# Fused top-32 attention and Mish feed-forward block on one core: another order of the work inside a slot on ScalarE and GpSimd, and the w_out split moved from slots 0 to 3 to slots 3 to 6

## The reference

```python
scores = q @ k.T / 8                       # per batch and head, 576 x 576
kth    = np.partition(scores, -32)[..., -32]
attn   = softmax(where(scores >= kth, scores, -1e9))
x      = (attn @ v) as 2304 x 512
h      = x @ w_in                          # 512 x 2048
g      = h * tanh(log1p(exp(h)))           # Mish
y      = g @ w_out                         # 2048 x 512
```

## Time and profile before

| | |
|---|---|
| median of 3 runs | 836.46 us (835.62 to 837.28) |
| profiled execution, its own time | 834.65 us |
| its span, first to last instruction | 832.9 us |
| mean granted TensorE clock | 0.975 of full |
| TensorE busy | 739.1 us (89%) |
| VectorE busy | 702.5 us (84%) |
| ScalarE busy | 557.2 us (67%) |
| GpSimd busy | 552.3 us (66%) |

### The profile page before, as it was taken

The page is one execution under the profiler, slowest core; times in us unless marked ns, Lnnn a source line. Parts: engine busy times, 40 slices in busy tenths (PEclk is TensorE's granted clock), DMA queues, the critical chain, the costliest instruction groups (busy, mean ns, idle before and its releaser), DMA issues.

```text
span 832.9 us, 16813 instructions
## 1 busy us (share of the span) xinstructions
PE 739.1 (89%) x6352; PEld 656.0 (79%) x6352; DVE 702.5 (84%) x1513; ACT 557.2 (67%) x994; POOL 552.3 (66%) x679
## 2 busy tenths in 40 slices
PE   2136787998999999999999999998999999999998
PEld 2125786887898888888888888888898888888896
DVE  5568999997999999989999999969999999996000
ACT  3456577686777686868686868685858686867330
POOL 3487556778676767787776767677676676767233
PEclk9995799999999999999999999999999999999999
DMA  7630000011020000111110000010110000000000
GB/s 225 241 106 7 7 11 4 20 43 42 14 71 8 21 15 16 27 41 48 39 35 8 20 8 23 14 48 8 36 51 18 10 21 7 17 1 14 2 13 25
DMA packets 27858, 28.87 MB, mean 35 GB/s; under 512 B 2433, under 2 KB 20865, under 8 KB 27265
## 3 DMA queue, kind: packets, MB, share of 16 engines
q1 hardware_dynamic: 27776, 27.80, 10.5%
HBM read 23.07 MB, written 4.72 MB: 33 GB/s over the span
## 4 chain that ended last, share of the span: by engine, by line
PE 61%; POOL 15%; ACT 9%; DVE 8%; issue 4%; DMA 2%; SPq 1%; ACTq 0%
PE ps_u L328 26%; PE ps_y L341 17%; POOL p_sb L564 7%; PE ps_s L289 7%; PE ps_o L312 6%; PE ps_s L275 5%; DVE left L507 3%; DVE top L515 3%; POOL w_lo L539 2%; ACT pT L419 2%; POOL g_lo L550 2%; ACT x_sb L394 2%; ACT p_sb L402 1%; DMA g_raw<-w_out 1%; POOL k_lo L528 1%
## 5 line engine op out<-in xcount | busy, mean ns | idle before, releaser
L515 DVE MAX8 top<-left 128x8 f32<-128x576 f32 x432 | 303.8, 745 | 0.0
L328 PE MATMUL ps_u<-xT,win 128*128 128x128 f32 x2304 | 280.2, 281 | 18.3 <-ACT xT L427 18.2
L328 PEld LDWEIGHTS ps_u<-xT,win 128*128 128x128 f32 x2304 | 267.9, 195 | 30.2 <-ACT xT L427 21.2
L564 POOL TENSOR_TENSOR p_sb<-x_sb,p_sb 128x576 f32<-128x576 f32 x144 | 201.7, 1423 | 84.5 <-ACT p_sb L402 84.4
L507 DVE MATCH_REPLACE8 left<-top,left 128x576 f32<-128x576 f32 x288 | 211.6, 742 | 0.0
L410 ACT ACTIVATE p_sb<-p_sb,neg_max 128x576 f32<-128x576 f32 x144 | 111.5, 774 | 84.4 <-POOL p_sb L564 84.2
L419 ACT ACTIVATE pT<-ps_s 128x640 f32<-128x640 f32 x144 | 93.8, 702 | 93.7 <-PE ps_s L289 93.2
L289 PE MATMUL ps_s<-ident,p_sb 128*128 128x128 f32 x720 | 95.3, 282 | 30.0 <-ACT x_sb L394 30.0
L341 PE MATMUL ps_y<-w_hi,g_hi 128*128 128x512 f32 x288 | 118.8, 412 | 0.7 <-ACT y_sb L450 0.7
L402 ACT ACTIVATE p_sb<-x_sb,limit 128x576 f32<-128x576 f32 x144 | 103.8, 775 | 22.8 <-POOL limit L555 22.8
L341 PE MATMUL ps_y<-w_hi,g_lo 128*128 128x512 f32 x288 | 112.6, 391 | 0.0
(11 more groups left out here) (38 smaller groups left out, 718.8 us busy)
## 6 DMA issues: line engine op xcount, KB each, us to landing
k_raw<-k_in SPq DMA_DIRECT2D x16, 288.0 KB, 3.2
q_raw<-q_in SPq DMA_DIRECT2D x64, 64.0 KB, 1.8
v_sb<-v_in SPq DMA_DIRECT2D x16, 256.0 KB, 2.9
win<-w_in SPq DMA_DIRECT2D x4, 1024.0 KB, 7.9
g_raw<-w_out SPq DMA_DIRECT2D x8, 512.0 KB, 3.8
y_out<-y_sb SPq DMA_DIRECT2D x16, 256.0 KB, 2.0
q_raw<-q_in SPq DMA_DIRECT2D x8, 128.0 KB, 2.0
v_sb<-v_in SPq DMA_DIRECT2D x16, 32.0 KB, 3.0
```

Of the source, the lines that this page charges most:

```text
L328: mm = pe.matmul(ps_u[:, n % 2, i, :], win[:, k, P * f:P * f + P], xT[:, k, :], start=(k == 0), stop=(k == KC - 1), skip_group_check=True)
L515: dve.max(best[:, t, EIGHT * r + EIGHT:EIGHT * r + 2 * EIGHT], left[:, t, :]).then_inc(found, 1)
L564: pool.tensor_tensor(p, x_sb[:, s % XS, t, :], p, ALU.subtract).then_inc(arg_ready, 1)
```

## The change

On ScalarE `copy_xT`, `copy_x` and `copy_y` go ahead of `exps` in a slot. On GpSimd the splits of keys and queries leave the end of slot s and go into slot s+1, behind `guard`, `negate` and `split_g` and ahead of `exponents`. The `w_out` split (ScalarE, GpSimd) and its loads (SyncE) move three slots later, to slots 3 to 6. Pairs 0 to 3 are split in slots -3, -2, -1 and 0, one a slot.

```diff
-WCHUNKS = 8
+WCHUNKS, WSLOT = 8, 3
...
-SPLIT_SLOT = {g: max(-3, g - 4) if g < PPB else LAST_USE[g - PPB] - 2 for g in range(PAIRS)}
+SPLIT_SLOT = {g: g - 3 if g < PPB else LAST_USE[g - PPB] - 2 for g in range(PAIRS)}
...
 # SyncE
-                if 1 <= s < WCHUNKS // 2:
-                    load_w(2 * s)
-                    load_w(2 * s + 1)
+                if 1 <= s - WSLOT < WCHUNKS // 2:
+                    load_w(2 * (s - WSLOT))
+                    load_w(2 * (s - WSLOT) + 1)
...
 # ScalarE
-                if 0 <= s - LAG_EXP < DUOS:
-                    exps(s - LAG_EXP)
-                m, j = divmod(s - DOWN_SLOT, GROUPS)
-                if m >= 0 and j == GROUPS - 1:
-                    copy_y(m)
                 if s >= LAG_PT and (s - LAG_PT) % PPB == PPB - 1:
                     copy_xT((s - LAG_PT) // PPB)
                 if 0 <= s + 2 < DUOS:
                     copy_x(s + 2)
+                m, j = divmod(s - DOWN_SLOT, GROUPS)
+                if m >= 0 and j == GROUPS - 1:
+                    copy_y(m)
+                if 0 <= s - LAG_EXP < DUOS:
+                    exps(s - LAG_EXP)
                 for g in splits_at(s):
                     split_k(g)
                 if s + 3 < DUOS:
                     split_q(s + 3)
-                if 0 <= s < WCHUNKS // 2:
-                    split_w(2 * s)
-                    split_w(2 * s + 1)
+                if 0 <= s - WSLOT < WCHUNKS // 2:
+                    split_w(2 * (s - WSLOT))
+                    split_w(2 * (s - WSLOT) + 1)
...
 # GpSimd
+            def splits(s):
+                for g in splits_at(s):
+                    split_k(g)
+                if s + 3 < DUOS:
+                    split_q(s + 3)
+
             for s in range(-3, DUOS + LAG_NORM):
+                if s == -2:
+                    splits(-3)
                 if 0 <= s - LAG_NORM:
                     guard(s - LAG_NORM)
                 if 0 <= s - LAG_EXP < DUOS:
...
                 m, j = divmod(s - MISH_SLOT - 1, GROUPS)
                 if m >= 0 and j < 2:
                     split_g(m, j)
+                if s > -2:
+                    splits(s - 1)
                 if 0 <= s - LAG_EXP < DUOS:
                     exponents(s - LAG_EXP)
                 if 0 <= s - LAG_NORM:
                     normalise(s - LAG_NORM)
-                for g in splits_at(s):
-                    split_k(g)
-                if s + 3 < DUOS:
-                    split_q(s + 3)
-                if 0 <= s < WCHUNKS // 2:
-                    split_w(2 * s)
-                    split_w(2 * s + 1)
+                if 0 <= s - WSLOT < WCHUNKS // 2:
+                    split_w(2 * (s - WSLOT))
+                    split_w(2 * (s - WSLOT) + 1)
```

## The result

The changed kernel takes 839.36 us (median of 6 runs, 838.77 to 840.6) against 835.66 us for the kernel before (6 runs, 833.73 to 837.28) on the same chips: a ratio of 1.0046, 95% interval 1.0031 to 1.0062. It is slower by half a per cent. The forecast was 833.8 us, range 823 to 841: the time lies in the range, on the other side of no change. The profiled execution took 840.6 us, the slowest of the six, with a span of 838.8 us, 5.9 more than before; between the medians it is 3.7.

The account below looks back on a forecast made before the run. VectorE was taken to bound up to slot 12, TensorE from there. 12.9 + 0.3 + 10.9 + 2.9 - 11.7 - 2.2 - 7.5 - 3.0 = 2.6 us gained: median 833.8 us, range 823 to 841.

Parts of the forecast that it names:

- Start, +12.9 and +0.3: Top-k start up to slot 8 gains 12.9 us; the road from limit(10) to TensorE's slot 12 gains 0.3.
- The ring of a slot with the w_out split: VectorE slot with w_out split, limit to next limit: 12.0 us taken; four such slots cost 7 us in all.
- The late load that I had priced: load_w queued behind a load_q waiting for the later q_lo; 0.8 us more for each slot it hits.
- xT, +10.9: TensorE's 0.9 us wait of up for xT goes in 12 slots from 18 to 66: 10.9 us gained.
- slot 70, +2.9: Wait for xT of 1.84 us and half clock behind it shrink to some 0.7: 2.9 us gained.
- q_lo in regular blocks, -11.7: Scores wait 0.58 and 0.48 us for q_lo behind split_g, 11 times in slots 19 to 68: 11.7 us lost.
- Slots with keys, -2.2 and -7.5: k_lo behind split_g delays q_lo: 2.2 us lost net in slots 30 to 32, 7.5 in the two mixed blocks.
- The clock, -3.0: TensorE falls to half clock after two of four new waits of 3.5 us or more: 3.0 us lost.
- rival B: Clock falls after all four long waits and in slot 11: 4.5 us more lost, 838.3 us; chance 0.22.
- C: Chain over mish, split_g and q_lo longer by 0.4 us in 28 slots: 11 us lost, 845 us; chance 0.20.
- D: ScalarE or GpSimd gets ahead, q_lo never late in regular blocks; the 11.7 us stay, 822 us; chance 0.10.

Follow-up runs that it names:

- the kernel with late keys: Changed kernel with splits of keys and queries ahead of split_g, but keys behind normalise in slots with s mod 4 = 0: 804.52 us, ratio 0.963.
- The filled kernel: Changed kernel with 15 to 30 transposes of the identity after values in slots 11, 15, 16, 31, 51 and 52: 833.66 us, ratio 0.9977.
- the kernel with GpSimd's old order: Changed kernel with GpSimd's splits back at the end of slot s, ScalarE's order new: 818.21 us, ratio 0.9797.
- the kernel with `q_lo` first: Changed kernel with GpSimd's splits of keys and queries moved ahead of split_g: 813.11 us, ratio 0.9728.

## Why the prediction was wrong

The forecast was 2.6 us of gain; between the profiled executions it is a loss of 5.9, so 8.5 are missing. The medians miss by less (839.4 for 833.8), since the profiled execution of the changed kernel is its slowest.

**Start, +12.9 and +0.3.** Right in kind; it gave 11.3 up to slot 8 and 9.6 up to slot 12. Two terms were mis-sized. The ring of a slot with the w_out split I put at 12.0 for all four; the later ones took 11.8, but the first took 14.3 (limit at 38.26, then at 52.56). Its scores, which ScalarE now awaits ahead of `exps`, came 3.0 us late; the later the load of queries shown above landed in the four profiles, the later slot 8 began. The late load that I had priced was one of w_out. So the stall came four times and not three in this execution; the kernel with late keys has three. And the road from top-k of slot 11 to slot 12 took 11.3 instead of 9.3: scores and `up` of slot 11 ran at half clock, 2.1 us. The filled kernel, where they do not, has slot 11 shorter by 0.7.

**xT, +10.9, and slot 70, +2.9.** Right: no wait for xT between slots 10 and 70, which gave 11.1, and slot 70 gave 2.8. Slots 14 and 50 gave 0.7 that I had not counted.

**q_lo in regular blocks, -11.7.** Right in place and mechanism. Slots with s mod 4 = 3 lost 0.58, as added up; those with s mod 4 = 0 lost 0.72 instead of 0.48. The 22 slots lost 14.1. Part of this is one gap that was too short: the table load ahead of `exps` starts only when `copy_y`, 0.61, has ended, where I had 0.48.

```profile
266.85 0.61 ACT L450 ACTIVATE y_sb<-ps_y 128x512 f32<-128x512 f32 x1
267.47 1.28 ACT L410 ACT_TABLE_LOAD   x1
```

**Slots with keys, -2.2 and -7.5.** The waits alone were near: 4.71 for 4.87 in slot 15, 2.35 for 2.55 in slot 31. Those of slots 16, 52 and 32 were smaller than forecast (2.56 and 2.64 for 3.55, 0.96 for 1.88), since half clock in `up` of the slot before runs while GpSimd works on. The filled kernel bears this out: with `up` at full clock, scores of slot 16 come 3.8 us late and those of slot 32 2.1.

**The clock, -3.0.** This is the step that failed, and it turned the sign. I took half clock for two of four long waits. It followed all four, and also the waits of slot 11, which only rival B had, and of slot 31, whose wait was forecast, but with no fall behind it. Scores and `up` in these six slots ran 11.5 us longer than at full clock: 2.1 in slot 11, 1.6 in 31, 2.5 and 1.5 in the first mixed block, 2.4 and 1.5 in the second (the 10.6 in the expectation above took 1.94 for scores at full clock, where it is 1.70). About 3 of these are given back by the smaller waits just named. Slots 15 to 17 thus cost 7.2 us against before, not 4.5, and slots 51 to 53 5.8, not 3.05 (the half clock of slot 53, 1.5, is gone, as forecast); slots 31 to 33 cost 2.9, not 2.2. The three numbers of the forecast leave out its 3.0 for the clock. So half clock cost about 8 us where 3.0 were allowed. The filled kernel shows the cause by experiment: 5.7 us back between medians, with 2.6 still lost in slot 32. That brings it to 0.9977 of the kernel before (0.9963 to 0.999), the side of the forecast. Since 1.2 us of the gain in its profile lie at the start, where nothing was changed, how much of the 5.7 is the clock stays open by about that.

Rival B had this mechanism and 838.3 us; I gave it 0.22. That the median of 839.4 is so close to it is in part luck: B prices neither slot 31 nor the shortfalls of the start and of `q_lo`, and between the profiled executions B, a loss of 1.9, is 4.0 short. My reason against it was that one of two waits of 2.58 had passed without a fall. It was a poor guide to the new waits: those of slots 16 and 52 are no longer than that (2.56 and 2.64) and were followed by half clock, and of two waits of 3.1 us in the kernel with GpSimd's old order one was not. What decides between them is not settled by these traces. The rule of the Trainium skill (TensorE: Matmul & The Clock Gate, HAM oscillation — how this bites in real kernels), that idle gaps let the clock fall again and a kernel pays at every one, agrees with the six long waits of the changed kernel; the wait of 3.08 us shows that not every one of such length is paid for.

**Rivals C and D.** C holds for 0.24 us in half of the regular slots, not for 0.4 in all: it is a small part of the loss. D did not happen: scores did wait for `q_lo`. With `q_lo` ahead of `split_g` the waits that D did away with are gone, and the time is 813.1 us.

## What to carry to other kernels

A step that moves earlier on one engine makes another later; ask of each consumer in the slot what its last input now stands behind. Here two reorders, each harmless or useful alone, closed a ring over three engines (copy, exp, table load, mish, cast, split, scores), and small splits (`q_lo`, 0.46 us, and in a few slots `k_lo`, 1.4 to 2.8) put ahead of a 3.5 us step instead of behind it were worth 26 us. When new waits of TensorE are forecast, let the range run from none to every long wait followed by half clock, and subtract what the next wait gives back; here the share taken from two earlier waits was far too low.

## What the runs showed of the hardware

In the changed kernel every wait of TensorE from 2.35 us up between slots 11 and 70 (slots 11, 15, 16, 31, 51, 52; in slots 11, 15, 31 and 51 it comes in two parts, taken together here) was followed by scores and `up` at half clock (1.2 instead of 2.4 GHz), while the 22 waits of 0.4 to 0.7 us and one of 0.96 us never were. Other kernels of this case show that the length alone does not decide: a wait of 2.01 us was followed by half clock, one of 3.08 us was not, and of three waits of 2.27 us (the kernel with `q_lo` first) two were. Where matmuls that compute nothing were put in a wait, scores and `up` behind them ran at full clock, and they paid for themselves: 5.7 us between medians, some 5 of them in the filled slots and behind.
